# Top-32 attention, an MLP and routed experts on one core: the masking and the small products move between engines, scores run a block ahead

## The reference

```python
# attention: batch 2, 8 heads, 576 positions, 64 wide
scores = scale * np.matmul(q, k.transpose(0, 1, 3, 2))
kth = np.partition(scores, -32, axis=-1)[..., -32:-31]
scores = np.where(scores >= kth, scores, -1e9)
attn = np.exp(scores - max);  attn /= sum(attn) + 1e-9;  x = attn @ v   # 1152 rows of 512
# MLP, 512 -> 2048 -> 512
h = x @ w_in;  x = (h * np.cos(h)) @ w_out
# 8 experts, 512 -> 1024 -> 512, 288 slots each, one expert per row
e = argmax(x @ w_gate);  the row takes the next free slot of e (or none)
out = gate_weight * (relu(slot_row @ w1[e]) @ w2[e])
```

## Time and profile before

| | |
|---|---|
| median of three runs | 697.26 us (696.23 to 697.46) |
| the profiled execution | 699.6 us, span 697.9 us |
| mean granted TensorE clock | 0.944 of full |
| busy in the span | PE 631.7, DVE 551.5, ACT 387.5, POOL 379.5 us |
| transfers | 68.58 MB, 98 GB/s over the span |
| w_out and w_in, 4096 KB each, issue to landing | 20.0 and 15.1 us |

### The profile page before, as it was taken

One profiled execution on the slowest core, in us unless ns is written; L12 is line 12 of the kernel. 1 busy time (PEld: TensorE's weight loads), 2 busy tenths in 40 slices (PEclk: granted clock), 3 DMA queues, 4 the chain that ended last, 5 costly groups with the idle time before them and its releaser, 6 DMA issues.

```text
span 697.9 us, 12783 instructions
## 1 busy us (share of the span) xinstructions
PE 631.7 (91%) x4180; PEld 544.3 (78%) x4180; DVE 551.5 (79%) x1009; ACT 387.5 (56%) x603; POOL 379.5 (54%) x278
## 2 busy tenths in 40 slices
PE   4678989999999999999999999989629999999996
PEld 2566977987987887888988979879528888888884
DVE  5999998989899799898899899315526667776673
ACT  2454675485585575675673863734406545556450
POOL 0779896589588688598696795940430111001111
PEclk9955797999999999999999999999859999999999
DMA  8697000000000000000000000050269455676510
GB/s 320 269 364 267 4 9 5 20 5 8 20 8 5 21 8 5 24 5 18 8 4 23 0 0 17 1 193 34 91 215 357 176 185 218 263 282 239 187 36 14
DMA packets 17789, 68.58 MB, mean 98 GB/s; under 512 B 1998, under 2 KB 6606, under 8 KB 15056
## 3 DMA queue, kind: packets, MB, share of 16 engines
q1 hardware_dynamic: 16000, 63.27, 24.0%
q0 software_dynamic: 1744, 4.73, 2.0%
HBM read 54.33 MB, written 14.45 MB: 99 GB/s over the span
## 4 chain that ended last, share of the span: by engine, by line
PE 54%; DVE 15%; issue 11%; POOL 10%; DMA 5%; ACT 4%; DVEq 0%; POOLq 0%; SPq 0%; ACTq 0%
PE p_o L1068 6%; DVE top L360 6%; PE p_a L1105 5%; DVE arena L363 5%; PE p_b L1105 4%; PE p_b L1133 4%; PE p_s L1034 4%; PE p_t L1050 3%; PE p_b L1134 3%; PE p_b L1135 3%; POOL mask L618 3%; POOL arena L622 2%; PE p_o L1288 2%; PE p_o L1290 2%; PE p_o L1289 2%
## 5 line engine op out<-in xcount | busy, mean ns | idle before, releaser
L360 DVE MAX8 top<-arena 128x8 f32<-128x576 f32 x288 | 203.8, 745 | 18.5 <-ACT arena L756 18.3
L363 DVE MATCH_REPLACE8 arena<-top,arena 128x576 f32<-128x576 f32 x216 | 158.5, 740 | 0.0
L618 POOL TENSOR_SCALAR mask<-arena,top 128x576 f32<-128x576 f32 x72 | 129.4, 1797 | 26.4 <-DVE top L360 19.0
L622 POOL TENSOR_TENSOR arena<-arena,mask 128x576 f32<-128x576 f32 x72 | 103.4, 1436 | 26.6 <-ACT arena L770 17.0
L1068 PEld LDWEIGHTS p_o<-arena,probsT 128*128 128x128 f32 x640 | 88.7, 213 | 15.0 <-ACT probsT L777 11.9
L1068 PE MATMUL p_o<-arena,probsT 128*128 128x65 f32 x640 | 90.7, 295 | 8.2 <-ACT probsT L777 8.2
L777 ACT COPY probsT<-p_t 128x640 f32<-128x640 f32 x72 | 50.4, 700 | 64.1 <-PE p_t L1050 63.9
L1050 PE MATMUL p_t<-ident,arena 128*128 128x128 f32 x360 | 59.2, 300 | 18.1 <-POOL arena L622 18.0
L1050 PEld LDWEIGHTS p_t<-ident,arena 128*128 128x128 f32 x360 | 44.8, 155 | 38.5 <-POOL arena L622 27.8
L756 ACT COPY arena<-p_s 128x576 f32<-128x576 f32 x72 | 44.2, 643 | 49.4 <-PE p_s L1034 49.4
L1034 PE MATMUL p_s<-arena,q_sb 64*128 64x224 f32 (+5 forms) x320 | 62.1, 495 | 7.2 <-DMA arena<-in_kt 4.5
(11 more groups left out here) (162 smaller groups left out, 1274.1 us busy)
## 6 DMA issues: line engine op xcount, KB each, us to landing
arena<-in_w SPq DMA_DIRECT2D x8, 2048.0 KB, 8.8
wff<-in_w SPq DMA_DIRECT2D x8, 2048.0 KB, 9.1
slot_rows<-y_now SPq DMA_DIRECT2D x1, 4626.0 KB, 27.0
wff<-in_w_out SPq DMA_DIRECT2D x1, 4096.0 KB, 20.0
wff<-in_w_in SPq DMA_DIRECT2D x1, 4096.0 KB, 15.1
wff<-slot_rows SPq DMA_DIRECT2D x8, 385.5 KB, 4.0
arena<-in_vones SPq DMA_DIRECT2D x2, 1300.0 KB, 9.5
q_sb<-in_q SPq DMA_DIRECT2D x36, 64.0 KB, 1.9
```

The lines of the kernel that those rows point to most:

```text
L360: nc.vector.max(best, src).then_inc(top_step, 1)
L363: nc.vector.match_replace(work[:, a, :], best, src, LOWEST).then_inc(top_step, 1)
L618: nc.gpsimd.tensor_scalar(mask[:], s_sb[:, t, :], top[:, t, TOP_K - 1:TOP_K], None, ALU.is_ge).then_inc(mask_made, 1)
L622: nc.gpsimd.tensor_tensor(probs[:, t % 2, :], probs[:, t % 2, :], mask[:], ALU.mult).then_inc(probs_ready, 1)
```

## The change

- The mask becomes a term that is subtracted before the exponential: GpSimd makes two biases per head (`bias`: -scale * max, and 2^80 * 32nd largest), ACT makes `pen` = relu(2^80 * (32nd largest - s)), GpSimd subtracts it from `s_sb` in place, and ACT's exp follows (`pens`, `mask_tile`, `exp_tile`). The compare, the product with the mask and ACT's own bias product go.
- VectorE in bodies does `pair_top` and `reciprocals` alone. GpSimd takes all four fractions, all low parts of g and of w_out. Sines, high and low parts go by single chunks.
- TensorE makes all scores of block i + 1 in body i, behind the transposes of heads 0, 2, 4, 6; those of block 0 come ahead of everything.
- SP issues w_out, w_in, v of batch 1 and k of batch 1 behind `next_queries(0)`, and `next_queries(1)` ahead of the two prefilling writes.
- In the tail, slots are computed ahead of gate weights, for the last block by fewer instructions; `low_w1(0, 0)` stands ahead of the last block's; the first `ranks` moves half a chunk ahead; TensorE gets 30 products of 512 columns into a bank that nobody reads, between the last count and the first expert.

```diff
 SP
+            sp.dma_start(vones[0], v_in[0]).then_inc(v_loaded[0], 16)
             next_queries(0)
+            sp.dma_start(w_out, w_out_d).then_inc(w_out_loaded, 16)
             sp.dma_start(w_in, w_in_d).then_inc(w_in_loaded, 16)
             sp.dma_start(wg[:], wg_d).then_inc(wg_loaded, 16)
+            sp.dma_start(vones[1], v_in[1]).then_inc(v_loaded[1], 16)
+            sp.dma_start(kT[:, 1], kt_in[:, 1]).then_inc(k_later_in, 16)
+            next_queries(1)
 VectorE, body
                 pair_top(i, 0)
+                if up and not down:
+                    reciprocals(i - 1)
+                pair_top(i, 1)
+                pair_top(i, 2)
                 if down:
-                    low_g(i - 2, 0)
-                    fraction(i - 2, 3, 2 * (i - 2) + 2, odd_turns_ready)
...
                     reciprocals(i - 1)
                 pair_top(i, 3)
 VectorE, tail
+            fraction(0)
+            choose_first()
+            fraction(1)
+            gated(0)
+            gated(1)
+            place_first()
+            low_g(0)
+            low_g(1)
+            fraction(2)
+            weigh_first()
+            gated(2)
+            fraction(3)
+            low_g(2)
+            gated(3)
+            low_g(3)
+            low_w1(0, 0)
+            place_last()
 GpSimd
+            def bias(i, p):
+                wait(pool, top_step, 56 * i + 14 * p + 14)
+                wait(pool, probs_ready, 8 * i + 2 * p - 6)
+                nc.gpsimd.tensor_tensor(biases[:, 2 * p:2 * p + 2, :], top[:, 2 * p:2 * p + 2, 0:TOP_K:TOP_K - 1],
+                                        signs[:].unsqueeze(1).broadcast_to([P, 2, 2]),
+                                        ALU.mult).then_inc(biases_ready, 1)
+            def mask_tile(i, t):
+                wait(pool, pen_ready, 8 * i + t + 1)
+                nc.gpsimd.tensor_tensor(s_sb[:, t, :], s_sb[:, t, :], pen[:, t % 2, :],
+                                        ALU.subtract).then_inc(masked, 1)
 GpSimd, first body: for p in 1, 2, 3
+                        bias(i, p)
+                        masks(i, p)
+                        low_w_out(2 * p - 2)
+                        low_w_out(2 * p - 1)
 GpSimd, bodies 2 to 8
+                normalise(i - 1)
+                masks(i, 2)
+                bias(i, 3)
+                fraction(i - 1, 0)
+                masks(i, 3)
+                fraction(i - 1, 1)
                 if more:
+                    bias(i + 1, 0)
                     masks(i + 1, 0)
+                gated(i - 1, 0)
+                gated(i - 1, 1)
+                low_g(i - 1, 0)
+                low_g(i - 1, 1)
+                if more:
+                    bias(i + 1, 1)
+                fraction(i - 1, 2)
+                fraction(i - 1, 3)
+                if more:
+                    mask_tile(i + 1, 2)
+                gated(i - 1, 2)
+                gated(i - 1, 3)
+                low_g(i - 1, 2)
+                low_g(i - 1, 3)
+                if more:
+                    mask_tile(i + 1, 3)
+                    bias(i + 1, 2)
 ACT
+            def pens(i, p):
+                wait(act, biases_ready, 4 * i + p + 1)
+                for t in (2 * p, 2 * p + 1):
+                    wait(act, masked, 8 * i + t - 1)
+                    nc.scalar.activation(pen[:, t % 2, :], s_sb[:, t, :], ACT.Relu, bias=biases[:, t, 1:2],
+                                         scale=-FAR).then_inc(pen_ready, 1)
 ACT, first body (scores(blk, p) copies a pair)
+                for p in range(1, H // 2):
+                    copy_pT(i, 2 * p - 2)
+                    scores(i + 1, p - 1)
+                    if p == 3:
+                        copy_o(i, 0)
+                    copy_pT(i, 2 * p - 1)
+                    pens(i, p)
+                    high_w_out(2 * p - 2)
+                    high_w_out(2 * p - 1)
+                    exps(i, p)
+                copy_pT(i, 6)
+                scores(i + 1, 3)
+                copy_pT(i, 7)
+                copy_o(i, 1)
+                pens(i + 1, 0)
+                high_w_out(6)
+                high_w_out(7)
+                exps(i + 1, 0)
 ACT, bodies 2 to 8, in this order
+  copy_pT(i, 0)  exp_tile(i, 2)  scores(i + 1, 0)  copy_pT(i, 1)  copy_xT(i - 1)  exp_tile(i, 3)  pens(i, 2)
+  copy_y(i - 2)  copy_pT(i, 2)  exp_tile(i, 4)  scores(i + 1, 1)  copy_h(i - 1, 0)  copy_pT(i, 3)
+  exp_tile(i, 5)  pens(i, 3)  copy_yT(i - 2)  copy_o(i, 0)  copy_h(i - 1, 1)  copy_pT(i, 4)  exp_tile(i, 6)
+  pens(i + 1, 0)  scores(i + 1, 2)  cosines(i - 1, 0)  copy_pT(i, 5)  high_g(i - 1, 0)  high_g(i - 1, 1)
+  copy_h(i - 1, 2)  exp_tile(i, 7)  copy_h(i - 1, 3)  copy_pT(i, 6)  exp_tile(i + 1, 0)  scores(i + 1, 3)
+  pens(i + 1, 1)  copy_logits(i - 2)  copy_pT(i, 7)  exp_tile(i + 1, 1)  cosines(i - 1, 1)  copy_o(i, 1)
+  high_g(i - 1, 2)  high_g(i - 1, 3)
 TensorE
-                    if t % 2 == 0 and t < LAG:
-                        scores(i, t // 2 + 2, keys)
-                    elif t % 2 == 0 and more:
-                        scores(i + 1, t // 2 - 2, next_keys)
                     transpose_probs(i, t)
+                    if t % 2 == 0 and more:
+                        scores(i + 1, t // 2, next_keys)
...
+            for n in range(IDLE_TURNS):    # 30
+                mm(p_t[:, 0:512], w_out_hi[:, 0, 0:P], w_out_hi[:, n % FC1, :], start=True, stop=True)
```

More of the change, by code:

```diff
@@ L483, in _ @@
             last = NBLK - 1
-            low_g(last - 1, 0)
-            fraction(last - 1, 3, 2 * last, odd_turns_ready)
             reciprocals(last)
@@ L840, in body @@
+            def body(i, up=True, down=True, mixed=False, batch=0, more=True):
+                first, second = not up, up and not down
+                if first:
+                    first_body(i)
+                    return
+                if second:
+                    second_body(i)
+                    return
                 copy_pT(i, 0)
-                scores(i, 5)
-                if up and not down:
-                    high_w_out(4)
+                exp_tile(i, 2)
+                if more:
+                    scores(i + 1, 0)
@@ L862, in body @@
-                if up:
-                    copy_h(i - 1, 0)
+                exp_tile(i, 4)
+                if more:
+                    scores(i + 1, 1)
+                copy_h(i - 1, 0)
                 copy_pT(i, 3)
+                exp_tile(i, 5)
+                pens(i, 3)
                 if down:
                     copy_yT(i - 2)
-                exps(i, 2)
                 copy_o(i, 0)
-                if up:
-                    copy_h(i - 1, 1)
+                copy_h(i - 1, 1)
+                copy_pT(i, 4)
@@ L872, in body @@
+                exp_tile(i, 6)
                 if more:
-                    scores(i + 1, 0)
-                    scores(i + 1, 1)
-                copy_pT(i, 4)
-                if up:
-                    cosine(i - 1, 0)
-                exps(i, 3, both=False)
-                exp_tile(i, 6)
-                if not up:
-                    high_w_out(1)
+                    pens(i + 1, 0)
+                    scores(i + 1, 2)
+                cosines(i - 1, 0)
                 copy_pT(i, 5)
-                if up:
-                    copy_h(i - 1, 2)
+                high_g(i - 1, 0)
@@ L913, in _ @@
+            for p in range(H // 2):
+                scores(0, p)
+            pens(0, 0)
             exps(0, 0)
```

458 lines of the change are left out of this document (229 added, 229 removed).

## The result

The changed kernel takes 707.56 us (median of 4 runs, 706.13 to 708.68); the kernel before, on the same chip, 697.36. The ratio is 1.0149, with a 95% interval of 1.0127 to 1.0171: slower by 10 us, where +7.4 (704 us) were forecast. The profiled execution took 708.68 us with a span of 706.9, 9.0 above that of before.

The account below looks back on a forecast made before the run. TensorE was taken as the bound, its steady blocks waiting 2.1 us, mostly for GpSimd's masks. 13.6 + 4.8 - 3.8 - 7.2 = +7.4 on 697.3 gave 704.7, written as 704; range 700 to 709, 8 in 10 within 688 to 713.

Parts of the forecast that it names:

- The opening: Start through block 2: longer pair loop, block 2 starting 7.8 us later, then 5.8 of waits there; +13.6 us.
- The reciprocals hold VectorE until 72: Block 1: VectorE's reciprocals make pair (1,1) ready at 82, so head (1,2) starts at 88.5 against 76.4.
- The clock's loss and gain: Opening: new gaps may drop TensorE's clock, while the earlier loss of 4.7 us is won back; taken to cancel.
- The blocks: Steady blocks 2 to 7: 47.3 plus 2.9 of waits make 50.2 us against 49.4; six blocks, +4.8.
- Chain (a): Steady block, head 5: ACT's copy_pT(5) comes late behind pens waiting for GpSimd's bias; TensorE waits 1.35 us.
- chain (c): Steady block, head 0: GpSimd's gated products and low_g(2) bring g_lo late; TensorE waits 1.3 us.
- Chain (b): Steady block: copy_h(3) comes 0.2 us late for down chunk 0.
- The last block: Block 8: two pairs of scores fewer and shrunken waits turn 46.5 into 42.7 us; -3.8 (-2 to -6).
- The tail: After the last block: earlier slots and sends bring the fetch of rows forward 7.1 us; in all -7.2 (-4 to -9).
- the win of 3.4: First expert phase, 12.0 us and half of it at the low clock, wins 3.4 us.
- The price of 3.3: Tail: the 30 idle matmuls end at 514 to 514.5, rows are there at 511; 3.3 us lost.
- relu brings no table load: ACT: Relu directly behind a Sin in block 1 could cost a load of 0 to 1.28 us; none counted.

Follow-up runs that it names:

- recip_later: Changed kernel with VectorE's reciprocals of block 0 moved behind the second pair of block 1 instead of the first; 707.49 us, ratio 1.0143.
- open_ahead: Changed kernel, opening reordered: w_out casts in ACT's gaps, Relus ahead of copy_pT, copy_o ahead of score copies, reciprocals behind block 1's second pair; 698.34 us, ratio 1.0008.
- best: open_ahead, vector_late_half, bias_ahead and swap_alone together, plus block 1 reordered on ACT and GpSimd, against the changed kernel; 665.94 us, ratio 0.9559.
- bias_ahead: Changed kernel with GpSimd working out bias(i+1, 0) ahead of fraction(i-1, 1) in blocks 2 to 8; 700.51 us, ratio 1.0041.
- vector_late_half: Changed kernel with VectorE taking back cosine products and low parts of the last two gated chunks from GpSimd, blocks 1 to 7; 694.71 us, ratio 0.9991.
- wout_in_gaps: Changed kernel with ACT's w_out casts moved behind copy_pT, ahead of score copies, the last two to block 1; 704.75 us, ratio 1.0114.
- swap_alone: Changed kernel with TensorE doing down chunk 2 of block 7 ahead of the transposes of the last x; 707.32 us, ratio 1.0143.
- best_order0: best with ACT's and VectorE's first two sums of the first expert, and the first's parts, ahead of the w2 split; 663.69 us, ratio 0.9509.
- w2_ahead: Changed kernel with SP issuing the first expert's w2 ahead of the wait for the last row send and of the row fetch; 711.18 us, ratio 1.0199.
- slots_late: Changed kernel with slots and weights of the first eight blocks worked out behind the low parts of the first expert's w1; 715.97 us, ratio 1.0281.

## Why the prediction was right, and where it was not

The sign and the mechanism were right: TensorE's copies stand on ACT behind waits for GpSimd. That 704 came within 3.6 us of 707.56 is in part luck. The stretches were off by -3.9 and -1.3 for the opening and the blocks, +4.7 and +2.0 for the last block and the tail, and these errors cancel to +1.5. The rest of the 3.6 is the rounding from 704.7 to 704 and the medians, which lie 10.2 apart where the spans of the traces lie 9.0 apart.

*The opening (13.6, and 0.8 for block 2; measured 10.5).* The chain was right head by head: a pair 11.88 (forecast 12.1), (1,0) 74.81 (76.5), (1,2) 84.68 (88.5), block 2 at 123.17 (127.5), where g_lo is 3.50 late (3.7) and the product 1.24 (2.1). Two steps were wrong. w_out was there at about 31 us and not at 33 to 34, so ACT never waited for it. And one step was wrong in its cause: "The reciprocals hold VectorE until 72, so pair (1,1) is ready at 82 and head (1,2) comes at 88.5." Both times of VectorE came true (70.89, 80.99), but (1,2) did not hang on them: recip_later takes the idle time away and moves nothing. It was the place of the Relus in ACT's stream, as open_ahead and best show. The clock's loss and gain did cancel, nearly: the wait of the earlier trace rows and the slow stretch behind it (4.7 us) went, and one came at 129.7 to 136.6, 6.9 us at a granted clock of 0.51, which by this is a loss of about 3.4 (an estimate).

*The blocks (+0.8 each).* 50.05 us against the 50.2 forecast; before it was 49.5. Chain (a), priced at 1.35, is 1.35 in bias_ahead; chain (c), priced at 1.3, is 1.47 in vector_late_half; with both mended a block takes 47.24, and 47.3 was worked out from the earlier trace rows. So these two waits were all that kept the block from TensorE's pace. Chain (b), put at 0.2 a block, shows once in the five blocks, as 0.27.

*The last block (-3.8; measured +0.9).* This is the step that failed. I let its waits shrink "to 1.1 (copy_h(3)) plus what VectorE's reciprocals take as before". The two old waits did go, but I left out chain (c) of my own list, at both of its ends. (The terms I named, 2.9 and 1.69 + 1.05 less 1.1, would even make -4.5.) At head 0, TensorE waits for g_lo for 2.86 us, not 1.3, since no scores of a next block stand in front of it there (in a steady block it waits 1.4, and a pair of scores takes 1.45), and here the clock falls behind it (to 437). After head 7 it waits 1.97 for x and 0.47 for g_lo:

```profile
433.08 0.50 PE L1220 MATMUL p_b<-w_out_lo,g_hi 128*128 128x512 f32 x1 [2.86 <-POOL g_lo L654]
...
476.99 0.66 PE L1170 MATMUL p_a<-ident,odd_whole 128*128 128x128 f32 x4 [1.97 <-DVE odd_whole L482]
478.12 0.79 PE L1220 MATMUL p_b<-w_out_lo,g_hi 128*128 128x512 f32 x1 [0.47 <-POOL g_lo L654]
```

(the rows are of the changed kernel's TensorE). vector_late_half takes 2.6 us off the block up to the transposes of x, of which some 1.5 are the clock: wout_in_gaps and bias_ahead have the same wait of 2.86, keep the full clock and take 45.9 us for it where the changed kernel takes 47.5. swap_alone shows that x and g_lo were late together. The scores that are not there, counted as a gain of 2.9, were also a cover.

*The tail (-7.2; measured -5.2).* The fetch came 7.0 us behind the logits (forecast 6.9), and the first slots at 499.4 (forecast 484 on the times of the kernel before, which is 498.2 here, as the last x comes 14.2 us later). Two parts were off. The last logits came 38.6 us behind the transposes of x and not 37.4, as slow down work follows the waits for x and g_lo. And the win of 3.4 in the first expert phase at full clock did not come: TensorE waits there for sums that wait for w2 (best_order0). The price of 3.3 for matmuls that overrun the rows was too high as well: they ended about when the rows landed, so that the two errors nearly cancel (+0.4).

*The rules of the Trainium skill.* That relu brings no table load (the Trainium skill, "ScalarE: Activation LUTs", Table sets: the hidden batching unit) holds here: in block 1 of open_ahead's trace the Relus start at 93.39, right behind the two sines that began at 92.33, with no load between. The lock of GpSimd and VectorE (the Trainium skill, "SBUF — State Buffer", Who interferes with whom) shows in the kernel before: there VectorE's two-input operation of 128x512, 0.69 us by itself, takes 0.87 to 1.68 in its 16 meetings with GpSimd, and 18 of the 72 compares meet a two-input operation of VectorE and take 2.01 on average, the other 54 1.73:

```profile
392.15 1.07 DVE L384 TENSOR_TENSOR turns<-turns,odd_whole 128x512 f32<-128x512 f32 x1
```
```profile
391.93 1.73 POOL L618 TENSOR_SCALAR mask<-arena,top 128x576 f32<-128x576 f32 x1 [0.21 <-POOL arena L622]
```

The operation that started second ended 0.44 us before the first one did, so by this profile it is a stretching, not a full wait for the other's end. In the changed kernel one meeting of this kind is left ahead of the sends, and it is in the block that failed: VectorE's division of the last x takes 1.47 us beside GpSimd's product and low part, and 0.69 in the kernel before and in vector_late_half, where GpSimd stands idle:

```profile
475.47 1.47 DVE L482 TENSOR_TENSOR odd_whole<-o_sb,rden 128x512 f32<-128x512 f32 x1
```

That is 0.8 of the 1.97 us that TensorE waits for x. vector_late_half is no test of the lock in the blocks: the added operations of VectorE fall where GpSimd is idle, or at the end of block 8 beside small ones.

## What to carry to other kernels

Before pricing a change that adds work, write each in-order engine's stream around the bottleneck's copies: what counts is which wait stands in front of a copy that TensorE wants, not how busy the engine is. Here 12 kernels with the same arithmetic ranged from 663.7 to 716.0 us through order and placement alone (medians). And treat edges (first and last trip of a loop) as their own stage: the work that is missing there was cover for a wait. And before a stretch of one trace is laid to an edit, look at the same stretch in traces where nothing in it was changed: here the opening differs by 5 us among them, block 8 by 1.6, the first expert phase by 2.

## What the runs showed of the hardware

- The send of the last block's rows lands in 2.9 us, and in 7.5 with a 2 MB transfer issued 2.2 us before it (w2_ahead).
- An operation of 128x512 with two inputs takes 0.69 us on VectorE and 1.27 on GpSimd (vector_late_half, means); one of 128x4 on GpSimd 0.20. Where they meet, both get longer: 0.87 to 1.68 and, for the compares, 2.01 for 1.73 (before).
- A send's issue on GpSimd beside VectorE's subtractions of w1 took 1.97 us at most (after), not the 4.98 of the earlier trace rows; in slots_late, beside none of them, seven of eight later ones take 0.98.
- TensorE often, not always, falls to the low clock behind waits of 2 to 3.5 us inside full work: a matmul of 512 columns takes 0.63 for 0.39 us (swap_alone), ten products 2.40 for 1.33 (after). Behind the wait of 2.86 us in block 8, the same in nine kernels' traces, the clock fell in seven (0.66 granted over the next 5 us in after) and stayed full in two (1.00 in wout_in_gaps and bias_ahead), which was worth 1.55 us.
